# Ninety matmuls over zeros ahead of a dense TensorE kernel, with the set-up work and six copies reordered

## The reference

```
X = fft(x, axis=1); X = fft(X, axis=2); x = X.real      # (4, 3008, 256) -> (12032, 256)
h = x @ w_in;  x = relu(h)**2 @ w_out                   # w_in (256, 2048), w_out (2048, 256)
h = x @ w2_in; out = (h * cos(h)) @ w2_out              # the same shapes
```

## Time and profile before

| | before |
|---|---|
| median of 3 timed runs | 1935.89 us (1935.87 to 1936.12) |
| the profiled execution: its own time / its span | 1935.89 us / 1933.9 us |
| PE busy | 1919.9 us (99%) in 8452 matmuls |
| LDWEIGHTS busy | 1589.3 us (82%) |
| DVE / ACT busy | 1431.7 us (74%) / 1260.3 us (65%) |
| first matmul | 9.92 us |
| chain that ended last | PE 98%, DMA 1%, DVE 1% |

### The profile page before, as it was taken

The page is one execution under the profiler, slowest core; times in us unless marked ns, Lnnn a source line. Parts: engine busy times, 40 slices in busy tenths (PEclk is TensorE's granted clock), DMA queues, the critical chain, the costliest instruction groups (busy, mean ns, idle before and its releaser), DMA issues.

```text
span 1933.9 us, 21334 instructions
## 1 busy us (share of the span) xinstructions
PE 1919.9 (99%) x8452; PEld 1589.3 (82%) x8452; DVE 1431.7 (74%) x1665; ACT 1260.3 (65%) x1320; POOL 0.2 (0%) x4
## 2 busy tenths in 40 slices
PE   7999999999999999999999999999999999999999
PEld 6888888888888888888888888888888888888887
DVE  8978767876876877777787687677677777777665
ACT  6867656765765765676675576576566667567555
POOL 0000000000000000000000000000000000000000
PEclk9999999999999999999999999999999999999999
DMA  7642112013112211100111311200000000000000
GB/s 280 244 146 81 52 59 84 29 36 129 56 41 91 74 52 67 54 6 22 33 39 36 110 55 52 91 31 6 11 22 6 11 22 6 1 22 1 1 11 22
DMA packets 37955, 105.82 MB, mean 55 GB/s; under 512 B 4312, under 2 KB 14808, under 8 KB 37600
## 3 DMA queue, kind: packets, MB, share of 16 engines
q1 hardware_dynamic: 35840, 90.53, 13.7%
q10 hardware_dynamic: 2016, 13.94, 2.1%
HBM read 85.91 MB, written 27.82 MB: 59 GB/s over the span
## 4 chain that ended last, share of the span: by engine, by line
PE 98%; DMA 1%; DVE 1%; ACT 0%; SPq 0%; issue 0%
PE ps L964 98%; DMA x<-x 1%; DMA ab<-scratch_a 0%; DMA scratch_a<-est 0%; PE ps L1115 0%; DVE kbuf L917 0%; DVE u L922 0%; SPq L361 0%; DVE pq L747 0%; PE ps L987 0%; DVE u L923 0%; DVE wsp L724 0%; DVE gh L882 0%; ACT u L690 0%; ACT gh L696 0%
## 5 line engine op out<-in xcount | busy, mean ns | idle before, releaser
L964 PE MATMUL ps<-gh,wo 128*128 128x502 f32 x4596 | 1119.0, 392 | 0.1
L964 PEld LDWEIGHTS ps<-gh,wo 128*128 128x128 f32 x4596 | 868.3, 189 | 188.5 <-DVE gh L882 1.0
L964 PE MATMUL ps<-y,wi 128*128 128x502 f32 x2304 | 555.0, 390 | 0.0
L964 PEld LDWEIGHTS ps<-y,wi 128*128 128x128 f32 x2304 | 434.2, 189 | 88.2
L929 DVE TENSOR_TENSOR u<-kbuf,ps 128x1004 f32<-128x1004 int32 x192 | 230.4, 1200 | 345.3 <-ACT kbuf L705 345.2
L882 DVE TENSOR_TENSOR gh<-u,gh 128x1004 fp32r<-128x1004 f32 x384 | 459.9, 1198 | 4.2 <-ACT u L697 2.1
L705 ACT ACTIVATE kbuf<-ps 128x1004 int32<-128x1004 f32 x192 | 193.7, 1009 | 348.3 <-PE ps L964 347.2
L690 ACT ACTIVATE u<-u 128x1004 f32<-128x1004 f32 x192 | 200.8, 1046 | 164.7 <-DVE u L923 164.5
L964 PE MATMUL ps<-eo,weo 128*128 128x502 f32 x1146 | 291.0, 389 | 0.0
L964 PEld LDWEIGHTS ps<-eo,weo 128*128 128x128 f32 x1146 | 215.6, 188 | 45.1 <-issue 0.2
L717 ACT ACTIVATE u<-u 128x1004 f32<-128x1004 f32 x192 | 200.4, 1044 | 65.2 <-DVE u L929 65.2
(11 more groups left out here) (93 smaller groups left out, 331.2 us busy)
## 6 DMA issues: line engine op xcount, KB each, us to landing
ring<-scratch_t SPq DMA_DIRECT2D x72, 378.0 KB, 4.0
xin<-x SPq DMA_DIRECT2D x36, 512.0 KB, 3.3
out<-osb SPq DMA_DIRECT2D x23, 502.0 KB, 3.6
scratch_t<-tables ACTq DMA_DIRECT2D x12, 756.0 KB, 4.6
raw<-scratch_eo SPq DMA_DIRECT2D x11, 502.0 KB, 5.0
scratch_eo<-est SPq DMA_DIRECT2D x14, 376.5 KB
stage_t<-tables SPq DMA_DIRECT2D x6, 756.0 KB, 16.1
tab_odd<-scratch_t ACTq DMA_DIRECT2D x2, 2268.0 KB, 11.5
```

The costliest lines, as they stand in the source:

```text
L964: op = pe.matmul(out_, a, b, start=start and i == 0, stop=stop and i == len(todo) - 1)
```

## The change

Four edits.

1. Ninety matmuls stand ahead of the first product on PE. Both operands are the 124 zero columns at the end of the tile `lastc` (124 weight columns, 124 moving columns, fp32r), and their result is overwritten by later work. They wait only for the first of the two memsets that write these zeros.
2. On ACT, `even_high(1)` moves behind `copy_w128(0)`, and `weo_high(1)`, `weo_high(2)` and `even_high(2)` move to other places among the `table_parts`.
3. On DVE, `w1_low(2)` moves ahead of `even_low(1)` and `fold_first(2)`. The low part of the last quarter of `w_in` was made in two halves, one ahead of `take_rows(2)` and one behind `finish_rows(2)`; it is now made in one piece, behind `finish_rows(2)`.
4. The six copies of the even table move from mix items 2 to 7 of tile 0 to its up items 10 to 15.

```
-ODD_COPIES, ODD_LOAD, EVEN_COPIES = range(2, 2 + 2 * KT), 9, range(2, 2 + 2 * KT)
+ODD_COPIES, ODD_LOAD, EVEN_COPIES = range(2, 2 + 2 * KT), 9, range(10, 10 + 2 * KT)
+WARM_UP = 90
...
         w1_high(1)
-        even_high(1)
         weo_high(0)
         w1_high(2)
         copy_w128(0)
+        even_high(1)
+        weo_high(1)
         table_parts(0)
-        weo_high(1)
+        weo_high(2)
+        even_high(2)
         table_parts(1)
-        even_high(2)
         table_parts(2)
-        weo_high(2)
         table_parts(3)
...
-            if (it.kind, it.t, it.sign) == ("mix", 0, 0) and it.index in EVEN_COPIES:
-                copy_tables(0, it.index - EVEN_COPIES.start)
+                elif it.index in EVEN_COPIES:
+                    copy_tables(0, it.index - EVEN_COPIES.start)
...
         fold_first(1)
+        w1_low(2)
         even_low(1)
         fold_first(2)
-        w1_low(2)
...
         finish_rows(1)
-        w1_last_low(0)
         take_rows(2)
...
         finish_rows(2)
-        w1_last_low(1).then_inc(wsp_lo, 1)
+        w1_low(3)
...
+        pe.wait_ge(zeroed, 1)
+        zeros = lastc[0][:, 4 * KT * B:]
+        for _ in range(WARM_UP):
+            pe.matmul(ps[0][0:P - B, 0, 0:P - B], zeros, zeros, start=True, stop=True)
         w1_product(0)
```

More of the change, by code:

```diff
@@ L725, in w1_low @@
                               ALU.subtract).then_inc(wsp_lo, 1)
[L727 to L731, removed]
         def weo_low(q):
```

## The result

The changed kernel takes 1946.65 us (median of 5, 1946.35 to 1947.51) against 1936.12 us (1935.87 to 1936.58): a ratio of 1.0055, 95% interval 1.0042 to 1.0069. It is slower, and it lies above 1945.0 us, the upper end of the range I gave. The profiled execution took 1946.74 us with a span of 1945.0 us.

What follows compares the result with a forecast made beforehand. PE was taken to bound the kernel: when it becomes dense, plus its work and gaps. Start +2.6 us and item 12's weight piece +0.9 gave +3.5 over 1935.89, so 1939.4 us; the range was 1936.0 to 1945.0 us.

Steps and rivals of the forecast that it cites:

- What bounds the kernel: PE's dense start plus its work plus gaps; a better start can give about 1.5 us for clock, 1 us of gaps.
- Edit 1: Ninety matmuls ahead of the first product: about 3 us at half clock, then 113 ns each, ending at 12.8 us.
- My own sign of being wrong: The ninety ending ahead of 10.4 or after 14 us, or item 12's gap over 2 us or missing.
- the clock never rises in them: Rival: the ninety stay at 1.2 GHz, 226 ns each, ending at 21.4 us; 1948.0 us, chance 0.07.
- the other side: Rival: load and matmul don't overlap in the ninety, 175 ns each, ending at 18.4 us; 1945.0 us, chance 0.17.
- Edits 2 and 3: New ACT and DVE order at the start: PE dense 2.1 + 0.53 = 2.6 us later, with the ninety ending at 12.8.
- the start costs (end - 10.2) us: Rule for the start: each 1 us by which the ninety end sooner or later shifts PE's dense moment by 1 us.
- the ninety fit: Rival: pace under about 90 ns, the ninety end by 10.4 us, start -0.1 us; 1936.7 us, chance 0.20.
- Edit 4: Moved copies delay item 12's weight piece: +0.9 us, ends 0 and 1.8; taking them from mix items gives 0.
- The sum: +2.6 us for the start, +0.9 for item 12's piece, 0 for the rest: +3.5, 1939.4 us; chance 0.50.

Runs made afterwards that it cites:

- the run with the wide matmuls: The changed kernel with 18 matmuls of 512 zero columns (124 weight columns) in place of the ninety: 1936.23 us (1.0002).

## Why the prediction was wrong

**What bounds the kernel** was right: PE is dense, the time follows the moment at which it becomes so, and every microsecond of the start came through to the end (11.0 at `kbuf`, 11.1 in the span).

**Edit 1 is the step that failed**, in the sentence "with about 3 us at half clock, as in the first product, the end is 1.1 + 3/2 + 90 x 0.113 = 12.8 us". The two paces were near: I took 226 and 113 ns, and the runs have 206 ns at half clock, and 114 ns at full clock with the same weight load. What was wrong is how long they run at half clock: not 3 us but all of it, 18.6 us, so that they ended at 19.6 us and not at 12.8. My own sign of being wrong was an end after 14 us. I took the 3 us from a product of 512 moving columns, and put them on matmuls of another shape. In the ninety one weight load follows the other every 206 ns, twice the 100 ns at which 124 columns stream with four weight columns. The runs with four weight columns and with 248 moving columns change one of the two each, and in both the clock rose; so did it over zeros. That the operands are zeros and that it is so early are excluded as causes; the shape is what is left.

The Trainium skill, TensorE: Matmul & The Clock Gate, Seeing it yourself, shows a stream of back-to-back matmuls that begins at the low clock and goes over to the high one inside the stream. The wide, the 248 column and the four column runs agree; the ninety, 18.6 us of them, do not.

**The rival "the clock never rises in them"** is what happened, and I gave it 0.07 and left its time out of the range. My reason against it, that the clock had risen with no more than matmuls in a row before it, treated all matmuls in a row as alike. Its price was 1948.0 us, 1.35 above the measured time. Two errors in it cancel in part: the pace was 206 and not 226 ns, -1.8 us, and I forgot that a clock that is still low behind the ninety makes the first product slow again, +1.5 us. The rival "the other side" has an end, 18.4 us, that is near the measured one, but by another cause: it put 175 ns on the pairs at full clock, and with this weight load and twice the moving columns they came every 114 ns there.

**Edits 2 and 3** held in the main. The rule "the start costs (end - 10.2) us" with the end at 19.6 gives 9.4, and 1.5 for the slow first product 10.9; the trace has 11.0 at `kbuf`. The fit is partly luck: the rule was made for a first product at full clock, and the slow one came on top. The places were right too: PE waits for the table piece ahead of step (0,1), and for `weo_low(0)` ahead of (1,0), and `w1_low(3)` in one piece takes 1.22 us of DVE behind the rows where 0.69 stood; `kbuf` is 0.4 us later by it, 0.53 was taken. In the rival "the ninety fit" I gave -0.1 us to the start; the run with the wide matmuls, where the first product is warm and in time, has `kbuf` at 34.52 against 34.89, -0.4.

**Edit 4** was right in its mechanism and mis-sized: 0.9 us taken, 0.4 to 0.5 measured in five profiles of eight and 1.1 to 1.4 in three, all within its ends of 0 and 1.8. Why some are twice the others is open. Taking the copies from the mix items could give nothing: PE has no gap there in either profile.

**The sum** with what was measured: 9.4 + 1.5 + 0.4 = 11.3 us over 1935.89, 1947.2; measured 1946.65, 10.5 over the runs beside it. The 0.5 to 0.8 us between them is not explained.

What stays open is by what mechanism these matmuls leave the clock low, since the runs only show which shapes did and which did not, and what the ninety would do over varied data. No run has the ninety's own shape at full clock, so the 113 ns that I took for it stays untested there.

## What to carry to other kernels

Matmuls put ahead to raise the clock are not all alike: with few moving columns and a full set of weight columns PE was busy in every row and stayed at 1.2 GHz. Read it from the durations of the weight loads (327 or 184 ns here), not from the busy share, and see that the matmuls end before the first real one can start. And before paying for a warm start, look at what PE would wait for next: here 1.5 us of clock were worth nothing that could be told in the old order and about 1 us by the medians in two new ones, because loads and the orders on ACT and DVE set the same moment.

## What the runs showed of the hardware

- A weight load of 124 columns in fp32r takes 327 ns at 1.2 GHz and 184 ns at 2.4 GHz; one follows the other every 203 to 206 ns and every 114 ns. With 4 weight columns, matmuls of 124 moving columns came every 100 and every 57 ns or so.
- 18.6 us of matmuls without a pause left the granted clock low, as the length of the product behind them shows; the page's clock row had 9 in all slices and its windows 1.00 there, before as after. For these first microseconds those figures can't be used. Later in an execution they can show a change: one profile has 0.50 from 11 to 14 us, where the first product is slow.
- 2.2 us without a matmul were enough in one execution for the clock to be low again; in another with 2.4 us it was still high at the first product.
